# A chunked delta-rule attention with a dense tail: solves as 32x32 tiles of the array, state updates as tiles of 32 and 16 columns, and the scaled v made by GpSimd

## The reference

```python
k_n = k / (np.linalg.norm(k, axis=-1, keepdims=True) + 1e-06)
for t in range(S):
    y[:, :, t] = np.einsum('bhd,bhde->bhe', q[:, :, t], state)
    v_old = np.einsum('bhde,bhd->bhe', state, kt)
    state = state + bt[:, :, :, None] * np.einsum('bhd,bhe->bhde', kt, vt - v_old)
```

## Time and profile before

| | |
|---|---|
| runs | 706.15 us median of 3 (699.31 to 708.35) |
| profiled execution | 708.49 us, span 706.8 us |
| busy in the span | PE 604.7 us, PEld 444.8, DVE 360.8, ACT 327.3, POOL 15.6 |
| mean granted TensorE clock | 0.833 of full speed |

### The profile page before, as it was taken

One profiled execution on the slowest core, in us unless ns is written; L12 is line 12 of the kernel. 1 busy time (PEld: TensorE's weight loads), 2 busy tenths in 40 slices (PEclk: granted clock), 3 DMA queues, 4 the chain that ended last, 5 costly groups with the idle time before them and its releaser, 6 DMA issues. The chain is left out here.

```text
span 706.8 us, 14724 instructions
## 1 busy us (share of the span) xinstructions
PE 604.7 (86%) x5784; PEld 444.8 (63%) x5784; DVE 360.8 (51%) x1139; ACT 327.3 (46%) x787; POOL 15.6 (2%) x28
## 2 busy tenths in 40 slices
PE   5469979969979987876868988668999999999998
PEld 4337657657757755654645733326878787878786
DVE  4985736735655654640001222565666565656563
ACT  1105546545644643653551211335555555565554
POOL 5000000000000000000000000000000000000000
PEclk9996757565675755755786999998999999999999
DMA  9212222231231012302359119910010101010101
GB/s 346 87 31 95 65 83 95 66 84 53 95 93 38 25 44 75 123 25 62 119 213 407 40 57 379 398 59 1 0 45 0 45 0 45 0 45 0 44 2 46
DMA packets 26922, 62.31 MB, mean 88 GB/s; under 512 B 2544, under 2 KB 13936, under 8 KB 26480
## 3 DMA queue, kind: packets, MB, share of 16 engines
q1 hardware_dynamic: 24224, 52.06, 21.1%
q10 hardware_dynamic: 2640, 9.44, 3.5%
HBM read 53.62 MB, written 4.72 MB: 83 GB/s over the span
## 5 line engine op out<-in xcount | busy, mean ns | idle before, releaser
L995 PE MATMUL acc<-g_h,wo_h 128*128 128x512 f32 x288 | 113.5, 394 | 5.4 <-DVE g_l L1048 3.4
L996 PE MATMUL acc<-g_h,wo_l 128*128 128x512 f32 x288 | 112.8, 392 | 0.0
L997 PE MATMUL acc<-g_l,wo_h 128*128 128x512 f32 x288 | 112.7, 391 | 0.0
L1048 DVE TENSOR_TENSOR g_l<-g,g_h 128x512 fp32r<-128x512 f32 x96 | 66.5, 693 | 72.6 <-ACT g_h L1016 72.6
L1016 ACT ACTIVATE g_h<-g 128x512 fp32r<-128x512 f32 x96 | 60.8, 633 | 79.0 <-DVE g L1045 79.0
L1045 DVE TENSOR_TENSOR g<-hp,sig 128x512 f32<-128x512 f32 x96 | 66.3, 691 | 19.0 <-ACT sig L1008 12.2
L471 DVE TENSOR_TENSOR tt<-tt,tmp 128x110 f32<-128x110 f32 (+35 forms) x366 | 74.8, 245 | 0.2
L466 DVE TENSOR_TENSOR tmp<-nm,tt 128x110 f32<-128x110 f32 (+35 forms) x366 | 74.6, 244 | 0.4
L257 PEld LDWEIGHTS rz_a<-rr,u 128*128 128x128 f32 x192 | 47.5, 332 | 36.3 <-DMA u<-dct 25.9
L257 PE MATMUL rz_a<-rr,u 128*128 128x48 f32 x192 | 51.0, 430 | 22.3 <-DMA u<-dct 22.3
L335 ACT ACTIVATE zb<-rz_a 32x192 f32<-32x192 f32 x96 | 30.9, 322 | 79.8 <-PE rz_a L257 79.0
(11 more groups left out here) (133 smaller groups left out, 674.3 us busy)
## 6 DMA issues: line engine op xcount, KB each, us to landing
kq<-in_kq_t SPq DMA_DIRECT2D x24, 512.0 KB, 4.3
ring<-in_w ACTq DMA_DIRECT2D x3, 2048.0 KB, 7.9
ring<-in_w SPq DMA_DIRECT2D x3, 2048.0 KB, 10.9
ring<-in_w SPq DMA_DIRECT2D x4, 1536.0 KB, 16.7
vn<-in_v_nat SPq DMA_DIRECT2D x24, 192.0 KB, 3.7
kn<-in_k_nat SPq DMA_DIRECT2D x24, 192.0 KB, 2.4
out_t<-res SPq DMA_DIRECT2D x18, 256.0 KB, 2.1
u<-dct SPq DMA_DIRECT2D x24, 128.0 KB, 2.7
```

What stands on the lines that cost most here:

```text
L995: eng.matmul(acc[d][:], wo_h[:, f, cols], g_h[:, f % R], start=(f == 0), stop=False)
L996: eng.matmul(acc[d][:], wo_l[:, f, cols], g_h[:, f % R], start=False, stop=False)
L997: i = eng.matmul(acc[d][:], wo_h[:, f, cols], g_l[:, f % R], start=False, stop=(f == NF - 1))
L1048: eng.tensor_tensor(g_l[:, f % R], g[:, f % R], g_h[:, f % R].bitcast(F32), ALU.subtract).then_inc(s_gl, 1)
```

## The change

1. The solve of one g is four matmuls of 32 rows and 32 columns, one for each quarter, with `dct` itself as weights. `u4`, its zeroing on POOL, the DMAs that fill it and the semaphore `s_u4` are gone. Whoever waited for `s_u4` now waits for DVE's `v_d` (the first solve of a round) or PE's `p_z` (the reuse of `dct`, and one weight slice).
2. The update of one g is two matmuls, on the state's rows 0 to 31 and 32 to 47, in place of one with 48 columns.
3. n V is one POOL operation for a chunk, in place of eight ACT operations. It is free to run as soon as the v rows and norms are there and the buffer of two chunks ago was read.
4. The order of arrays in SBUF is another, with 320 spare floats, so that what the weight slices overlay fits the new waits.

```diff
@@ sync
-            def spread_u(r):
-                for q in range(HG):
-                    eng.dma_start(u4[r % 2][quarter(q), :, q], dct[r % 2][quarter(q)]).then_inc(s_u4[r % 2], DMA)
...
-                if c % CR == CR - 1 and r + 1 < NR:
-                    eng.wait_ge(v_d, r + 2)
-                    if r:
-                        eng.wait_ge(p_z, 2 * CR * r)
-                    spread_u(r + 1)
@@ gpsimd
-            for t in u4:
-                eng.memset(t[:], 0.0).then_inc(z_u4, 1)
-            for r in range(2, NR):
-
-                eng.wait_ge(v_d, r - 1)
-                eng.memset(tt[r % 2][:], 0.0).then_inc(z_tt, 1)
+            for c in range(NCH):
+                r = c // CR
+
+                eng.wait_ge(s_vn[c % 3], DMA * (c // 3 + 1))
+                eng.wait_ge(v_n, r + 1)
+                if c >= 2:
+                    eng.wait_ge(v_r, 2 * c - 2)
+                u = NG * (c % CR)
+                eng.tensor_tensor(nv[:, c % 2], vn[:, c % 3], nn[:, r % 3, u:u + NG].unsqueeze(2).broadcast_to([P, NG, D]),
+                                  ALU.mult).then_inc(g_nv, 1)
+                if c % CR == 0 and 2 <= r + 2 < NR:
+
+                    eng.wait_ge(v_d, r + 1)
+                    eng.memset(tt[r % 2][:], 0.0).then_inc(z_tt, 1)
@@ tensor
             def solve(c, half):
+
                 r = c // CR
                 if c % CR == 0 and half == 0:
-                    eng.wait_ge(s_u4[r % 2], HG * DMA * (r // 2 + 1))
+                    eng.wait_ge(v_d, r + 1)
                 eng.wait_ge(v_r, 2 * c + half + 1)
                 for gi in range(GH):
                     g = GH * half + gi
-                    i = eng.matmul(rz[half][:, D * (GH + gi):D * (GH + gi) + D],
-                                   u4[r % 2][:, c % CR, :, :, g].rearrange("p q t -> p (q t)"), rr[:, g],
-                                   start=True, stop=True, skip_group_check=True)
+                    for q in range(HG):
+                        i = eng.matmul(rz[half][quarter(q), D * (GH + gi):D * (GH + gi) + D],
+                                       dct[r % 2][quarter(q), c % CR, :, g], rr[quarter(q), g],
+                                       start=True, stop=True, skip_group_check=True)
                 i.then_inc(p_z, 1)
...
                 for b in HALVES[half]:
-                    for a in range(2):
-                        g, at = 2 * b + a, HG * D * (b % 2)
-                        i = eng.matmul(sp[half][64 * a:64 * a + D, at:at + HG * D], kn[:, c % 3, g],
-                                       zb[:, g].rearrange("p q e -> p (q e)"), start=False, stop=True, skip_group_check=True)
+                    for lo, hi in ((0, 32), (32, D)):
+                        for a in range(2):
+                            g, at = 2 * b + a, HG * D * (b % 2)
+                            i = eng.matmul(sp[half][64 * a + lo:64 * a + hi, at:at + HG * D], kn[:, c % 3, g, lo:hi],
+                                           zb[:, g].rearrange("p q e -> p (q e)"), start=False, stop=True,
+                                           skip_group_check=True)
                 i.then_inc(p_s, 1)
@@ scalar
-                if c + 1 < NCH:
-                    scale_v(c + 1)
                 z_out(c, 1)
                 s_out(c, 1)
```

More of the change, by code:

```diff
@@ L89, in attention @@
         gc = sb("gc", [P, 2, CR, NG, C])
-        dct = two("dct", [P, CR, C, NG])
-        u4 = two("u4_", [P, CR, HG, C, NG])
+        dct = [sb("dct0", [P, CR, C, NG])]
+        beta = sb("beta", [P, NR, C])
+        tmp = sb("tmp", [P, 2, 9 * 16])
+        small = {n: sb(n, [P, C]) for n in ("nsq", "rt", "n1", "n2", "n3", "cb", "cneg")}
+        sb("spare", [P, 320])
+        dct.append(sb("dct1", [P, CR, C, NG]))
         pd = sb("pd", [P, PR, NG, C])
@@ L98, in attention @@
         zb = sb("zb", [P, NG, HG, D])
-        beta = sb("beta", [P, NR, C])
-        tmp = sb("tmp", [P, 2, 9 * 16])
         mask = sb("mask", [P, C])
         nn = sb("nn", [P, 3, C])
-        small = {n: sb(n, [P, C]) for n in ("nsq", "rt", "n1", "n2", "n3", "cb", "cneg")}
         rz = [bank("rz_a", [P, 512]), bank("rz_b", [P, 512])]
@@ L113, in attention @@
         s_vn = [sem(f"s_vn{i}") for i in range(3)]
-        s_u4 = [sem(f"s_u4{i}") for i in range(2)]
         s_beta = sem("s_beta")
-        z_s, z_zb, z_u4, z_tt = (sem(n) for n in ("z_s", "z_zb", "z_u4", "z_tt"))
+        z_s, z_zb, z_tt = (sem(n) for n in ("z_s", "z_zb", "z_tt"))
         s_pool = sem("s_pool")
@@ L122, in attention @@
         p_g0, p_g, p_k, p_q, p_z, p_s, p_y = (sem(n) for n in ("p_g0", "p_g", "p_k", "p_q", "p_z", "p_s", "p_y"))
-        a_gk, a_nv, a_z, a_s, a_y, a_rt = (sem(n) for n in ("a_gk", "a_nv", "a_z", "a_s", "a_y", "a_rt"))
+        a_gk, a_z, a_s, a_y, a_rt = (sem(n) for n in ("a_gk", "a_z", "a_s", "a_y", "a_rt"))
+        g_nv = sem("g_nv")
         v_p, v_r, v_t, v_nsq, v_n, v_d, v_c = (sem(n) for n in ("v_p", "v_r", "v_t", "v_nsq", "v_n", "v_d", "v_c"))
@@ L164, in _ @@
                 load_kq(c)
-            eng.wait_ge(z_u4, 2)
-            eng.wait_ge(v_d, 1)
-            spread_u(0)
             for c in range(NCH):
-                r = c // CR
                 if c + QR < NCH:
@@ L174, in _ @@
                 if c + 3 < NCH:
-                    eng.wait_ge(a_nv, c + 1)
+                    eng.wait_ge(g_nv, c + 1)
                     load_vn(c + 3)
@@ L313, in gram_out @@
                 eng.activation(gc[:, r % 2, c % CR], gp[c % 2][:, :, 0:C], ACT.Copy).then_inc(a_gk, 1)
[L315 to L325, removed]
             def z_out(c, half):
@@ L363, in _ @@
                 gram_out(c)
-            scale_v(0)
             root(1)
@@ L388, in _ @@
                     load_slice(eng, 3)
-                    eng.wait_ge(s_u4[(NR - 1) % 2], HG * DMA * ((NR - 1) // 2 + 1))
-                    eng.wait_ge(s_u4[(NR - 2) % 2], HG * DMA * ((NR - 2) // 2 + 1))
+                    eng.wait_ge(p_z, 2 * CR * (NR - 1))
                     load_slice(eng, 4)
@@ L445, in scales @@
                 if r >= 3:
-                    eng.wait_ge(a_nv, CR * (r - 2))
+                    eng.wait_ge(g_nv, CR * (r - 2))
                 eng.transpose(nn[:, r % 3], n3[:]).then_inc(v_n, 1)
@@ L477, in inverted @@
                 if r >= 2:
-                    eng.wait_ge(s_u4[r % 2], HG * DMA * (r // 2))
+                    eng.wait_ge(p_z, 2 * CR * (r - 1))
                 eng.transpose(dct[r % 2][:].rearrange("p c i g -> p i c g"), tt[r % 2][:]).then_inc(v_d, 1)
```

## The result

The changed kernel takes **587.5 us** (median of 4 runs, 586.4 to 592.0) against 706.9 before (699.3 to 708.4): ratio 0.834, 95% interval 0.827 to 0.840. The profiled execution took 592.0 us, span 590.2.

The account below looks back on a forecast made before the run. The prediction took PE's own order in the chunks as the bound, with a DMA wait and long solves visible in it. Its terms, 61 + 22 + 11 + 5 - 5 = 94 us off 708.5, gave 614 us, range 594 to 650.

Parts of the forecast that it names:

- the clock: PE's granted clock in the chunks: no net effect on the time, taken as 0 and +-15 us.
- signs of being wrong: What would refute the forecast: a solve over 1.4 us, or the clock staying at its lower level.
- Solves: PE's 48 solves in the chunks: 0.85 us each instead of 2.12, all on the path, saving 61 us.
- DMA wait: PE's six waits for the DMAs that spread the inverse go, saving 22 us, at least 16.
- n V off ACT: ACT takes z of half 1 sooner, so PE waits less for `zb`: 11 us saved, bounds 5 and 14.
- Update: PE's hand-overs around the update overlap more when all are 32 wide: 5 us saved, bounds 0 and 10.
- Given back: PE waits for right sides after ACT's root, and DVE's lumps cost something: -5 us, bounds 0 and -24.
- A: Rival: a solve's four row tiles on PE stream in turn, 2.4 us a solve in the mean; 683 us, chance 0.10.
- B: Rival: each solve tile on PE waits for the last to drain, 4.5 us a solve; 785 us, chance 0.03.
- C: Rival: n V on POOL holds DVE still, DVE becomes the bound, chunks take 10.2 us or so; 632 us, chance 0.07.

Follow-up runs that it names:

- nowait128: The changed kernel with the earlier 128x128 solves, their weight array filled once, so no DMA wait after the first round: 650.4 us, ratio 0.924.
- wide128: nowait128 with each solve matmul streaming 128 moving columns in place of 48: 628.4 us, ratio 0.895.
- rest_only: The kernel before with only n V on POOL and the narrow updates, keeping its 128x128 solves and their DMA wait: 679.8 us, ratio 0.963.
- no_elim: update48 without DVE's elimination in rounds 1 to 5: 574.5 us, ratio 0.817.
- update48: The changed kernel with its updates 48 columns wide again: 586.9 us, ratio 0.8335.
- act_nv: The changed kernel with n V back on ACT as eight operations between the halves: 630.6 us, ratio 0.894.
- wait32: The changed kernel with the inverse's DMAs kept, into an unread array, and each round's first solve waiting for them: 609.8 us, ratio 0.868.
- contig48: update48 with the inverse transposed so that a tile's 32 weight columns are neighbours: 587.3 us, ratio 0.834.

## Why the prediction was wrong

The solves, the waits and n V gave time in the way that the prediction has it, and the sum of 94 us came out as 119. The step that failed is **the clock, "I take 0 and +-15 us"**; beside it the term of n V was too small and that of the update was nothing. The signs of being wrong that the prediction names, a slow solve and a low clock, did not come: it had none for a kernel faster than its range.

- **The clock.** At equal solves it is worth 22.0 us between 0.81 and 0.99 (nowait128, wide128), 12 us for each tenth of the mean. From 0.68 to 0.90 that makes, as an estimate, 27 us, and 25 were missing. A second reading: wide128 has everything of the change but the short solve, terms that sum to 33 us, and is 76 us faster than the kernel before; the 43 more go with a clock of 0.99 for 0.68, which by the same price are 38. I had weighed only idle time and the size of tiles. The evidence stood in front of me: a solve's loads lasted the same at both clocks, so PE was "busy" 2.1 us and streamed 8 records of 48 columns. I priced what that took and not what it did to the clock of everything else. My price (0.4 us a chunk for ten points of the time at the higher level) was high, 0.25 by the runs, but the share moved by over 40 points where I allowed some 16.
- **Solves, 61 us.** Duration forecast 0.85, measured 0.71 and 0.87. In the time: 62.9 us from nowait128 to the changed kernel. That it agrees is partly luck: by way of wide128, 22 of it are the clock, and from there a solve shorter by 1.46 us (70 us for 48) shows up as 41, not all of it on the path as the prediction has it. DVE, late in some chunks now, takes a part of the rest; how much isn't measured with long solves. The cause of the length was mis-named: not "loading 128 columns" but their stride.
- **DMA wait, 22 us.** 22.3 with short solves, 29.3 with long ones (rest_only to nowait128), where the mean clock rises with it, 0.74 to 0.81.
- **n V off ACT, 11 us.** 43 as the last step. I wrote that the old order would cost more with the short solve, and then added a term from the old chunk to a solve term "all of it on the path". Only one order of the parts can be summed. With n V moved first it is 25 (rest_only, if the updates are nothing there too), then the DMA wait 29, then the solve 63: 117.6 us. At 12 us for a tenth of the clock, an estimate again, 7, 8 and 11 of these are the clock; what is left, 18, 21 and 52, stands against a forecast of 11 (n V, update and what is given back), 22 and 61. With n V last, the chunk of 10.2 us had swallowed part of the solves' gain; that this is the whole surplus of the 43 isn't shown.
- **Update, 5 us.** 0. The hand-over from update to pz does overlap more (0.17 us in the rows above, 0.08 before), but twice the instructions came with it, and that these cost what it gave is argued, not shown. In one of the changed kernel's updates PE stands 1.9 us with nothing to wait for, and what follows runs at the lower clock:

```profile
105.55 0.52 PE L270 MATMUL sp_b<-zb,kn 128*32 128x192 f32 x7 [0.39 <-ACT zb L325]
107.95 0.65 PE L270 MATMUL sp_b<-zb,kn 128*16 128x192 f32 x9 [1.88 <-issue]
108.30 1.46 PE L280 MATMUL yp<-zb,pd 128*32 128x192 f32 x16
109.69 0.87 PE L256 MATMUL rz_a<-rr,dct 32*32 32x48 f32 x32
```

- **Given back, -5 us.** The elimination costs 12.5 us now (no_elim). A faster clock speeds PE and leaves DVE where it was.
- **Rivals.** A and B are refuted: a solve would take 1.6 us at the higher clock by A and 4.5 in the mix of clocks by B, and it takes 0.71 and 0.87. The Trainium skill's rule for A (TensorEngine Tiling (Array Packing), "Gotcha 1: PSUM Pressure") doesn't hold here, where the four row tiles write four different quarters of the partitions of one bank; the trace decides. C happens in part: n V takes 0.83 us on POOL (my bounds 0.36 and 1.1), and one pair of DVE's elimination operations that meets it took 1.04 us instead of 0.43. But the gain is 25 us above the forecast even with it.

What stays open: why PE stands in the midst of its groups (I take it for the supply of instructions, since it grew from nothing to 35 us as each solve went from 8 to 96 records, but no run isolates it), and what the clock is worth with short solves, since its price was measured only with long ones. It may be less there: two executions of the changed kernel took 587.5 us both, at mean clocks of 0.950 and 0.965, and update48, at 0.98 in its chunks for 0.91, takes the same time.

## What to carry to other kernels

A phase in which TensorE is busy but streams few columns has a second price: the clock of all the work around it. So have stands: behind those of 2.1 us in act_nv and of 5 us in wait32 the groups ran at the lower clock. Look for groups whose duration doesn't change with the granted clock; ask first for the stride of their weights, then for a denser form. Sum the parts of a change in one order, re-reading who is late after each; and where the clock is under 1, give its rise a term of its own.

## What the runs showed of the hardware

- Weight loads of 128 float32 columns 32 bytes apart follow each other at 0.24 us, neighbouring ones at 0.12, both on PE that is otherwise the same. The Trainium skill (TensorE: Matmul & The Clock Gate, "LDWEIGHTS") gives the load by the number of columns alone; an estimate from its formula is 0.107 us for 128. The neighbours are near it and the strided ones, at over twice that, aren't.
- More streaming in the same time made the kernel faster: 650.4 to 628.4 us, with the clock of the chunks at 0.99 for 0.81.
- Four tiles of 32 rows and 32 columns, with their outputs in four different quarters of the partitions of one PSUM bank, work at once: 32 records of 48 columns in 0.71 us, where in turn they would take some 1.6.
- POOL's n V can starve. Of the 24, three took 3.5 to 4.7 us instead of 0.83 while DVE ran two-input operations back to back; nobody waited for them, since each has a chunk of time. The longest:

```profile
173.50 4.71 POOL L193 TENSOR_TENSOR nv<-vn,nn 128x384 f32<-128x384 f32 x1 [7.63 <-DVE rr L396]
```

- DVE's blockwise transpose of 1024 elements takes 1.25 us when it writes runs of 8 neighbours and 1.93 when it writes elements 128 bytes apart (update48, contig48).
